# A capacity-limited expert search in which the next phase's keys are prepared inside the search

## What is computed

```python
cap = N // E                                  # 4352 // 8 = 544
logits = x @ w_gate
order = np.argsort(-logits.flatten())
for idx in order:
    tok, e = (int(idx) // E, int(idx) % E)
    if assigned[tok] >= 0 or counts[e] >= cap:
        continue
    assigned[tok] = e
    counts[e] += 1
for e in range(E):
    mask = assigned == e
    h = np.maximum(x[mask] @ w1[e], 0.0)
    out[mask] = h @ w2[e]
```

## Time and profile before

| | us |
|---|---|
| median of 3 runs (lowest, highest) | 390.84 (390.67, 391.18) |
| the profiled execution | 390.38 |
| its span | 388.7 |
| VectorE busy, share of the span | 228.6 (59%) |
| TensorE matmul busy | 313.4 (81%) |
| ScalarE busy | 90.9 (23%) |
| first `best` of the search (phase 0) | at 75.4 |
| phases 2 to 6, each | 31.4 |
| mean granted TensorE clock | 0.906 of full speed |

### The profile page before, as it was taken

The page is one execution under the profiler, slowest core; times in us unless marked ns, Lnnn a source line. Parts: engine busy times, 40 slices in busy tenths (PEclk is TensorE's granted clock), DMA queues, the critical chain, the costliest instruction groups (busy, mean ns, idle before and its releaser), DMA issues.

```text
span 388.7 us, 7717 instructions
## 1 busy us (share of the span) xinstructions
PE 313.4 (81%) x2591; PEld 225.7 (58%) x2591; DVE 228.6 (59%) x873; ACT 90.9 (23%) x189; POOL 86.5 (22%) x105
## 2 busy tenths in 40 slices
PE   6999999233134789879888888988989999999986
PEld 4799999222023556646555565655667686755552
...
PEclk9799999755555599999999999999999999899999
...
DMA packets 50182, 31.59 MB, mean 81 GB/s; under 512 B 9072, under 2 KB 47600, under 8 KB 50160
## 3 DMA queue, kind: packets, MB, share of 16 engines
...
...
## 4 chain that ended last, share of the span: by engine, by line
PE 53%; DVE 29%; issue 8%; DMA 3%; POOL 2%; ACT 2%; SPq 1%; DVEq 0%; ACTq 0%; POOLq 0%
PE psum L508 14%; PE psum L516 9%; DVE feats L1049 5%; DVE feats L1007 4%; PE psum L418 4%; PE psum L405 4%; PE psum L481 4%; PE psum L389 2%; PE psum L745 2%; PE psum L468 2%; PE psum L602 2%; PE psum L596 2%; PE psum L560 2%; PE psum L610 1%; PE psum L534 1%
## 5 line engine op out<-in xcount | busy, mean ns | idle before, releaser
L508 PE MATMUL psum<-kq_sb 128*128 128x272 f32 x256 | 82.8, 434 | 1.1 <-ACT kq_sb L787 0.8
L516 PE MATMUL psum<-v_flat,kq_sb 128*128 128x272 f32 x256 | 77.0, 408 | 0.4 <-ACT v_flat L794 0.4
L357 POOL DMA_INDIRECT kq_sb<-x_by_token,tokens x40 | 38.2, 955 | 154.7 <-DVE tokens L1016 137.4
L794 ACT ACTIVATE v_flat<-psum 128x544 f32<-128x544 f32 x64 | 39.8, 624 | 136.4 <-PE psum L508 136.4
L367 POOL DMA_INDIRECT slot_logits_by_token<-kq_sb,tokens x40 | 41.6, 1040 | 60.4 <-ACT kq_sb L806 50.6
L516 PEld LDWEIGHTS psum<-v_flat,kq_sb 128*128 128x128 f32 x256 | 45.3, 191 | 9.7 <-ACT v_flat L794 3.1
L508 PEld LDWEIGHTS psum<-kq_sb 128*128 128x128 f32 x256 | 44.6, 196 | 8.9 <-ACT kq_sb L787 1.4
L596 PE MATMUL psum<-mask_pad,feats 128*128 128x32 bf16 (+1 forms) x490 | 23.9, 179 | 24.8 <-DVE feats L1049 24.0
L1049 DVE TENSOR_TENSOR feats<-digit_pad,steps 128x640 bf16<-128x640 int16 (+1 forms) x84 | 42.2, 544 | 0.4
L596 PEld LDWEIGHTS psum<-mask_pad,feats 128*128 128x128 bf16 x490 | 18.8, 99 | 34.9 <-issue 13.8
L890 DVE TENSOR_TENSOR feats<-ab 128x2048 f32<-128x2048 f32 (+1 forms) x10 | 19.6, 1964 | 16.3 <-ACT ab L757 9.0
...
## 6 DMA issues: line engine op xcount, KB each, us to landing
...
kq_sb<-w SPq DMA_DIRECT2D x128, 64.0 KB, 1.9
...
kq_sb<-x_by_token,tokens POOLq DMA_INDIRECT x40, 2.6
```

What stands on the lines that cost most here:

```text
L357: pool.indirect_dma_start(out=xg[0:rows, b, :], out_offset=None, in_=x_dram, in_offset=bass.IndirectOffsetOnAxis(ap=tokens[0:rows, which, ...
L508: mm = pe.matmul(psum[:, 2 + 2 * (f % 2) + half, 0:HALF], w1_sb[:, f * P:(f + 1) * P], xsT[:, half * HALF:(half + 1) * HALF], start=True, ...
L516: mm = pe.matmul(psum[:, 6 + half, 0:HALF], w2_sb[:, f, :], hT[:, f % 2, half * HALF:(half + 1) * HALF], start=f == 0, stop=f == CHUNKS - 1)
L794: act.activation(hT[:, f % 2].rearrange("p (b t) -> p b t", b=2), psum[:, 2 + 2 * (f % 2):4 + 2 * (f % 2), 0:HALF], ACT.Relu)\
```

## The change

**The second choice is prepared during the search.** `current` holds for every token three numbers: the two halves of the key and the label. While a phase searches, the same three for the token's best other open expert are worked out in `second` (with `L` less the expert that the token points at), and then the difference `change`. Once it is known which expert is full, tokens that point at it get `current + change` (`moved`). `key`, the reduce for `best` and the label reduce at a phase's start are gone; the closed expert's logits are lowered in `L` at level 0.

**The steps stand in three places of each level**, on VectorE: `while_partial` (after the thresholds, while TensorE counts), `while_counts` (after the copy of the partial sum) and `while_digit` (after the flags). Listing is spread over the same places, the one-hot compare in four pieces of 32 rows. `list_members` stands after level 2's digit, `keep_list` in level 3.

**Which expert is full and how many are missing** comes from flags kept of all levels (`flags`), summed by six small matmuls, and from the row of counts above the digit (`above_row`). The totals with `chosen` and `row_totals` are gone. `minus_cap` is one row, written from the same counts.

**TensorE's order:** three products instead of two behind each digit but the last; neither ahead of the last level's digit nor between it and `LAST` is there one; `outputs` before the ties' matmuls; the ranks after level 0's partial sums; no warm-up matmuls in the phases. The first half of the next phase's thresholds stands before the wait for the ties, the second behind the mask.

The tail and the network are the same. The core of the diff:

```diff
-            WHILE_FLAGS = [1, 1, 1, 1, 1, 1]
-            WHILE_DIGIT = [2, 2, 2, 2, 2, 2]
-            WHILE_TOTALS = 2
-            LAST = len(PRODUCTS) - FIRST - sum(WHILE_COPY) - sum(WHILE_FLAGS) - sum(WHILE_DIGIT) - WHILE_TOTALS
+            WHILE_FLAGS = [1, 1, 1, 1, 1, 0]
+            WHILE_DIGIT = [3, 3, 3, 3, 3, 0]
...
-                if listing:
-                    rank_members(i - 1, 0)
...
+                    if listing and l == 0:
+                        rank_members(i - 1, 0)
...
+                    if l == LEVELS - 1:
+                        for d in range(LEVELS - 1):
+                            pe.matmul(psum[:, 1, METS:METS + EXPERTS + 1], ones_b[0:2 ** DIGITS[d], :],
+                                      flags[0:2 ** DIGITS[d], d, :], start=d == 0, stop=False)
...
-                    pe.matmul(psum[:, 0, 0:1], ones_b[0:J, :], full[0:J, :], start=True, stop=True)\
-                        .then_inc(S["digit_ready"], 1)
+                    if l == LEVELS - 1:
+                        pe.matmul(psum[:, 1, METS:METS + EXPERTS + 1], ones_b[0:J, :], flags[0:J, l, :],
+                                  start=False, stop=True)
+                    pe.matmul(psum[:, 0, DIG:DIG + 1], ones_b[0:J, :], flags[0:J, l, EXPERTS:EXPERTS + 1],
+                              start=True, stop=True).then_inc(S["digit_ready"], 1)
                     fill(WHILE_DIGIT[l])
-                    if listing and l == 3:
+                    if listing and l == 2:
                         list_members(i - 1)
-                pe.wait_ge(S["chosen_ready"], i + 1)
-                pe.matmul(psum[:, 0, 0:2 * EXPERTS], ones_b[:], minus_caps[:], start=True, stop=False)
-                pe.matmul(psum[:, 0, 0:2 * EXPERTS], ones_b[:], row_totals[:], start=False, stop=True)\
-                    .then_inc(S["totals_ready"], 1)
-                fill(WHILE_TOTALS)
+                fill(LAST)
+                if network:
+                    outputs(i - 2)
                 pe.wait_ge(S["tie_ready"], i + 1)
                 pe.matmul(psum[:, 1, 0:TILES], before[:], tie[:], start=True, stop=True)
                 pe.matmul(psum[:, 1, TILES:2 * TILES], ones_b[:], tie[:], start=True, stop=True)\
                     .then_inc(S["tieranks_ready"], 1)
-                fill(LAST)
-                if network:
-                    outputs(i - 2)
-                    keep_warm(7, 0)
+                pe.wait_ge(S["above_row_ready"], i + 1)
+                pe.matmul(psum[:, 0, BASE:BASE + EXPERTS], ones_h[0:J, :], above_row[0:J, :], start=True, stop=True)\
+                    .then_inc(S["base_ready"], 1)
                 if listing:
                     turn_rows(i - 1)
-                if network:
-                    keep_warm(7, 3)
...
+            def key_halves(target):
+                n = did(dve.tensor_scalar(sign[:], best[:].bitcast(I32), 31, -2 ** 31, ALU.arith_shift_right,
+                                          ALU.bitwise_or))
+                after(n)
+                after(did(dve.tensor_tensor(sign[:], sign[:], best[:].bitcast(I32), ALU.bitwise_xor)))
+                did(dve.tensor_scalar(halves_i[:, 0], sign[:].bitcast(U32), 16, None, ALU.logical_shift_right))
+                after(did(dve.tensor_scalar(halves_i[:, 1], sign[:].bitcast(U32), 0xFFFF, None, ALU.bitwise_and)))
+                after(did(dve.tensor_copy(halves[:], halves_i[:])))
+                return did(dve.tensor_scalar(target[:, 0:2], halves[:], 2.0 ** -SHIFTS[0], None, ALU.mult))
+            def first_digit():
+                after(did(dve.tensor_scalar(digit, current[:, 0], TO_FLOOR0, None, ALU.add)))
...
+            def while_partial(i, l, listing, network):
+                after(count[0])
+                if l == 0 and listing:
+                    after(did(dve.tensor_tensor(L[:], L[:], closed[:].unsqueeze(2).to_broadcast(wide), ALU.add)))
+                if l == 1 and listing:
+                    did(spread(0, 32))
+                if l == 2 and listing:
+                    spread(96, P).then_inc(S["onehot_ready"], 1)
+                if l == 3:
+                    if network:
+                        after(did(dve.tensor_copy(tokens[:, 4, :], tokens[:, 1, :])))
+                    if listing:
+                        keep_list(i - 1, 1)
+                if l == 4:
+                    did(dve.tensor_tensor(is_rank[:], is_best[:], rankx[:], ALU.mult))
+                if l == 5:
+                    key_halves(second)
+                    if network:
+                        dve.wait_ge(S["l2_sent"], i - 1)
+                        did(dve.tensor_copy(tokens[:, 0, :], tokens[:, 4, :]))
+            def while_counts(i, l, listing, network):
+                after(count[0])
+                if l == 0 and listing:
+                    dve.wait_ge(S["ranks_ready"], i)
+                    places_of_blocks()
+                if l == 1 and listing:
+                    did(spread(32, 64))
+                if l == 2:
+                    did(dve.scalar_tensor_tensor(out=e3[:], in0=mask, scalar=-BIG, in1=L[:], op0=ALU.mult,
+                                                 op1=ALU.add))
+                if l == 3:
+                    did(dve.tensor_reduce(best[:], e3[:].rearrange("p e c -> p c e"), AX.X, ALU.max))
+                if l == 4:
+                    did(dve.tensor_reduce(second[:, 2], is_rank[:].rearrange("p e c -> p c e"), AX.X, ALU.max))
+                if l == 5:
+                    did(dve.tensor_tensor(change[:], second[:], current[:], ALU.subtract))
+            def while_digit(i, l, listing, network):
+                after(count[0])
+                if l == 0 and listing:
+                    places_in_blocks(0)
+                if l == 1 and listing:
+                    did(spread(64, 96))
+                if l == 3:
+                    did(dve.tensor_tensor(is_best[:], e3[:], by_token(best), ALU.is_equal))
...
-                after(did(dve.tensor_reduce(best[:], L[:].rearrange("p e c -> p c e"), AX.X, ALU.max)))
...
-                n_label = did(dve.tensor_reduce(label[:], is_best[:].rearrange("p e c -> p c e"), AX.X, ALU.max))
...
-                after(did(dve.tensor_tensor(chosen[:], over[:].unsqueeze(2).to_broadcast([P, 2, EXPERTS, TILES]),
-                                            mask.unsqueeze(1).to_broadcast([P, 2, EXPERTS, TILES]), ALU.mult)))
-                with nc.allow_low_precision("a partition's TILES tokens: exact in bfloat16"):
-                    dve.tensor_reduce(row_totals[:], chosen[:], AX.X, ALU.add).then_inc(S["chosen_ready"], 1)
...
+                n_full = did(dve.scalar_tensor_tensor(out=fullw[:], in0=psum[:, 1, METS:METS + EXPERTS],
+                                                      scalar=psum[:, 1, METS + EXPERTS:METS + EXPERTS + 1],
+                                                      in1=rankw[:], op0=ALU.is_ge, op1=ALU.mult))
+                n_at = did(dve.tensor_scalar(at[:], now, digit_found, None, ALU.is_equal))
+                after(n_full)
+                n_fw = did(dve.tensor_reduce(fw[:], fullw[:], AX.X, ALU.max))
+                did(dve.tensor_scalar(over[:], now, digit_found, None, ALU.is_gt))
+                after(n_fw)
                 dve.scalar_tensor_tensor(out=tie[:], in0=label[:], scalar=fw[:], in1=at[:], op0=ALU.is_equal,
                                          op1=ALU.mult).then_inc(S["tie_ready"], 1)
-                after(did(dve.tensor_scalar(nfull[:], rankw[:], fw[:], -1.0, ALU.is_equal, ALU.mult)))
...
+                dve.scalar_tensor_tensor(out=above_row[0:J], in0=part_idf[0:J].to_broadcast([J, EXPERTS]),
+                                         scalar=psum[0:J, 0, DIG:DIG + 1], in1=psum[0:J, 0, 0:EXPERTS], op0=ALU.is_equal,
+                                         op1=ALU.mult).then_inc(S["above_row_ready"], 1)
+                n = did(dve.scalar_tensor_tensor(out=moved[:], in0=label[:].unsqueeze(1).to_broadcast([P, 3, TILES]),
+                                                 scalar=fw[:], in1=change[:], op0=ALU.is_equal, op1=ALU.mult))
+                did(dve.tensor_copy(label_was[:], label[:]))
+                did(dve.tensor_scalar(nfull[:], rankw[:], fw[:], -1.0, ALU.is_equal, ALU.mult))
+                after(n)
+                after(did(dve.tensor_tensor(current[:], current[:], moved[:], ALU.add)))
+                first_digit()
+                thresholds(0, 0)
+                dve.wait_ge(S["tieranks_ready"], i + 1)
+                n = did(dve.tensor_tensor_scan(colsum[:, 1:TILES + 1], ones_row[:], psum[:, 1, TILES:2 * TILES], 0.0,
+                                               ALU.mult, ALU.add))
+                dve.wait_ge(S["base_ready"], i + 1)
+                did(dve.scalar_tensor_tensor(out=need8[:], in0=psum[:, 0, BASE:BASE + EXPERTS], scalar=1.0,
+                                             in1=nfull[:], op0=ALU.mult, op1=ALU.mult, accum_out=need[:]))
+                after(n)
```

(25 more changed lines are left out.)

183 lines of the change are left out of this document (78 added, 105 removed).

## The result

| | us |
|---|---|
| changed kernel, median of 4 runs (lowest, highest) | 401.59 (400.79, 402.54) |
| kernel before, the same chip, 4 runs | 390.99 (390.67, 391.18) |
| ratio, with its 95% interval | 1.0287 (1.0262 to 1.0313) |
| profiled execution of the changed kernel, its span | 402.26, 400.5 |
| mean granted clock, before and after | 0.906 and 0.863 |

The forecast was 379.8, faster. The kernel became slower by 10.6 us, on the other side.

What follows compares the result with a forecast made beforehand. No engine is full; the search hands values between VectorE and TensorE, and serial VectorE work after the last digit is attacked. Phase 2 -2.4, phases 3 to 6 4 x -1.9, after phase 6 -1.1: total -11.1, 379.8 us, range 375.5 to 385.5.

Steps and rivals of the forecast that it cites:

- I cost their loss at nothing: Phase's end on TensorE: removed keep-warm matmuls stood in the wait for ScalarE's copy of the rows, so cost 0.
- rival (3): Phase's end: TensorE falls to 1.2 GHz with fewer fillers and bunched waits; +2.7 in each of five, 393 us; chance 0.03.
- D5 to P0: From VectorE's first read of the last level's digit to the next level 0's copy `partial`: 8.15 us instead of 11.47.
- the tail: After phase 6: the first product waits for `member`, near 6.5 us after the last digit's read instead of 7.6; -1.1.
- From the search's end to P0: Last digit to next level 0's `partial`: TensorE's path counts, VectorE waits 1.2 us for it; -3.3 a phase.
- The cover: VectorE's new steps in each level hide in idle gaps of 0.38 us (before `flag`) and 0.60 (before digit), or behind products.
- Rival (1): Levels' new VectorE steps delay flag and digit by full length, 2.4 us a phase; time 397 us; chance 0.05.
- the mark: Sign of a wrong forecast: flag starting over 0.9 us after the copy `partial` in levels 2 to 4.
- level 0: From its copy `partial` to its digit's first read: 1.9 us, as `places` overruns the gaps; +0.4 a phase.
- level 3: List matmuls move here behind three products: 2.75 us from level 2's digit to its `partial` against 2.03; level's term +0.95.
- level 5: Unhidden `key_halves` makes level 4's digit to `partial` 2.45 us (+0.8), `partial` to digit 1.1 (-0.43); term +0.35.
- Phase 1: Its last digit stays near 122.80 us; earlier token list and turned rows shift phase 2's first `partial` to 131.5, -3.85.

Runs made afterwards that it cites:

- e3: Changed kernel with the three warm-up matmuls of before put back behind the turned rows: 388.75 us, ratio 0.9987 to the kernel before.
- e9: Changed kernel with three unused matmuls in each of three TensorE waits (before last level's counts, before `outputs`, behind turned rows): 381.12 us, ratio 0.9774.
- e4: Kernel before with only the change's placing of products, its warm-up matmuls kept: 402.88 us, ratio 1.0341.
- e6: Changed kernel with unused matmuls before `outputs`, behind the turned rows, and in phase 1: 384.35 us, ratio 0.9823.
- e10: As e7, with one product moved from ahead of the token list to level 1's digit: 374.52 us, ratio 0.9614 to the kernel before.
- e2: Changed kernel with three unused matmuls only in the wait before `outputs`: 384.95 us, ratio 0.9896 to the kernel before.
- e7: As e6, with four products instead of six ahead of level 0, two moved behind the digits of levels 0 and 4: 375.49 us, ratio 0.9643.

## Why the prediction was wrong

**The step that failed** is the sentence "I cost their loss at nothing", on the three warm-up matmuls, and with it rival (3), which got 0.03: the clock was taken to hold at the phase's end. In its place the granted clock was at half for 10.2 us behind each of phases 2 to 6, 4.2 us of time in each stretch from D5 to P0. With the three matmuls put back (e3) the ratio is 0.9987 instead of 1.0287; with all three waits filled (e9) it is 0.9774. The mechanism of rival (3) is the one that happened. The evidence that I set against it was wrong: I took products packed earlier as speaking for the clock, and e4 shows that packing them earlier empties the phase's end (+13.7 us by itself in the kernel before). I had listed the places where VectorE's new steps need cover and not the places where TensorE's clock needs it, though the diff showed four of five products and three fillers leaving one stretch.

**Its size** was short too. I priced turned rows to P0 at half clock, +2.7; the trace has 168.64 - 161.04 = 7.60 against 4.93 in e9, 2.67. But the clock is down from `outputs` on: 1.5 more in each phase, and 3.1 in the tail, which I left out (D5 of phase 6 to the span's end 107.9, in e9 104.8). Between the spans of the changed kernel and e9, 400.5 and 379.4, lie 4 x 4.2 = 16.8 behind phases 2 to 5, 0.3 behind phase 1, 3.1 in the tail, and 1.0 by which the start of the search differed, with no edit there: 21.2, and the spans differ by 21.1. (The first P0 lies anywhere from 79.5 to 82.6 in the profiles of the changed kernel's variants, so a microsecond there is chance.)

**The rest of the sum** can be read from the changed kernel and from e9, whose clock held. D5 as in the prediction, us:

| (before: first `over`; else `fullw`) | before | predicted | changed | e9 |
|---|---|---|---|---|
| D5 of phase 0 | 94.80 | 97.45 | 99.99 | 98.95 |
| D5 of phase 1 | 122.80 | 122.8 | 125.68 | 124.62 |
| P0 of phase 2 | 135.33 | 131.5 | 134.48 | 133.09 |
| a network phase | 31.42 | 29.5 | 34.1 | 29.90 |
| of it, D5 to P0 | 11.47 | 8.15 | 12.4 | 8.20 |
| of it, P0 to D5 | 19.95 | 21.4 | 21.7 | 21.7 |
| D5 of phase 6 to the span's end | 107.7 | 106.6 | 107.9 | 104.8 |

- *From the search's end to P0* was right, term by term, in e9: `outputs` 1.24 after D5 (1.3), the turned rows 2.03 behind it (1.94), the first product 1.60 on (1.61), the products 2.91 (2.92). VectorE of e9, the end of the stretch:

```profile
191.27 0.44 DVE L1065 TENSOR_TENSOR L<-L,closed 128x272 f32<-128x272 f32 x1
193.07 0.19 DVE L1138 CAST partial<-psum 128x32 f16<-128x32 f32 x1 [1.36 <-PE psum L601]
```

  Its last step ends at 191.71, D5 + 6.84 (6.9), and it idles 1.36 (1.2).
- *The cover.* Rival (1) didn't happen: the reduce of level 3 delays the flags to P3 + 0.66, under the 0.9 that I had named as the mark, and TensorE's product hides it. In the changed kernel, phase 3, with the forecast in brackets: level 0, P0 to D0 1.75 (1.9); level 3, D2 to P3 2.81 (2.75), waiting 0.79 for the list; level 5, D4 to P5 2.56 (2.45) and P5 to D5 1.24 (1.1). Together P0 to D5 was 0.3 longer than forecast. So the Trainium skill's advice to minimize VectorE's operations (VectorE: DVE Perf Modes, "Rules for kernel authors") didn't decide here: e9 has 100 of them in a phase instead of 94 and is 2.3% faster than the kernel before. Steps that don't wait for the one ahead follow it closely (`best` 0.10 behind `partial`, 181.30 to 181.40).
- *Phase 1* was off. D5 came at 125.68 and not near 122.8: the start and phase 0 cost 5.2 (99.99 - 94.80) instead of 2.65, of which 1.0 is the difference that e9 doesn't have. The turned rows stand at 126.79, D5 + 1.11 (forecast 1.05), and from them to P0 of phase 2 it is 7.69 at half clock (7.65 in the forecast). So both steps behind D5 were right, and the shift of P0 of phase 2 was -0.85 in place of -3.85 (-2.2 in e9) because D5 was late. The token list came at 116.83, 2.3 earlier than before and not 4.8; this didn't matter, as TensorE waited for the ties (0.94 us) and not for the rows.
- *The tail* gained 2.9 in e9, where 1.1 was forecast. The kernel before has a stretch at half clock in its tail, from 328.9 to 332.3 (the 8 in its clock line), and e9 has none. Among the changed kernel's variants, which share the tail's code, e6, e9 and e10 have no stretch at half clock in it and take 104.7 to 104.8 from D5 of phase 6; e2 and e7, with one of 3.4 us, take 106.4 and 106.3. So about 1.5 of the 2.9 is the clock, and the rest is near the forecast. The prediction had read this stretch of the line as full speed.

With these misses of both signs e9, the change with its clock kept, comes to 381.1; the forecast was 379.8. That they lie so near is in part luck: P0 of phase 2 came 1.6 later than forecast and the phases from there to the last D5 took 2.1 more, but the tail took 1.8 less, most of it by a fall of the clock that e9 was spared.
